# An expert tile computed at the end of attention, from counts over the first eight token tiles

## The reference

```python
def _attn_ref(q, k, v, i_gate, f_gate, o_gate):      # (4, 8, 768, 40): batch, heads, tokens, head dim
    for t in range(S):
        m_new = np.maximum(f_gate[:, :, t] + m, i_gate[:, :, t])
        f_stab, i_stab = np.exp(f_gate[:, :, t] + m - m_new), np.exp(i_gate[:, :, t] - m_new)
        m = m_new
        C = f_stab * C + i_stab * outer(v_t, k_t)
        n = f_stab * n + i_stab * k_t
        y[:, :, t] = sigmoid(o_t) * (C @ q_t) / np.maximum(np.abs(n . q_t), 1.0)

def _moe_ref(x, w_gate, w1, w2):                     # x (3072, 320); 8 experts, 320 -> 1024 -> 320
    logits = x @ w_gate
    expert_idx = np.argmax(logits, axis=1)
    gate_w = softmax(logits)[expert_idx]
    for e in range(E):
        mask = expert_idx == e
        out[mask] = gate_w[mask, None] * (np.maximum(x[mask] @ w1[e], 0.0) @ w2[e])

def _moe2_ref(x, phi, w1, w2):                       # soft mixture: 8 experts with 4 slots each
    logits = x @ phi
    slot_input = softmax(logits, over tokens).T @ x
    slot_out[e] = np.maximum(slot_input[e] @ w1[e], 0.0) @ w2[e]
    return softmax(logits, over slots) @ slot_out
```

## Time and profile before

| | |
|---|---|
| median of 3 runs | 543.53 us (543.01 to 544.75) |
| the profiled execution | 541.98 us |
| its span, first to last instruction | 540.2 us |
| mean granted TensorE clock | 0.953 of full |
| busy: TensorE, weight loads | 490.0 us (91%), 415.7 us (77%) |
| busy: VectorE, ScalarE, GpSimd | 285.9, 196.3, 327.5 us |
| DMA | 86.51 MB, 160 GB/s over the span |

### The profile page before, as it was taken

One profiled execution on the slowest core, in us unless ns is written; L12 is line 12 of the kernel. 1 busy time (PEld: TensorE's weight loads), 2 busy tenths in 40 slices (PEclk: granted clock), 3 DMA queues, 4 the chain that ended last, 5 costly groups with the idle time before them and its releaser, 6 DMA issues.

```text
span 540.2 us, 11228 instructions
## 1 busy us (share of the span) xinstructions
PE 490.0 (91%) x3957; PEld 415.7 (77%) x3957; DVE 285.9 (53%) x589; ACT 196.3 (36%) x427; POOL 327.5 (61%) x303
## 2 busy tenths in 40 slices
PE   6698999999984188999999999999999999999983
PEld 5587888888873077898989889898988988887231
DVE  7866777867784876633434444334344344334024
ACT  2544464545651402333233333233242323331013
POOL 3687878777696044569796978888098525112100
PEclk9778999989998579999999999999999999999997
DMA  8058788877930023345170505060091282106928
GB/s 226 5 166 273 268 278 254 260 245 222 304 129 36 2 71 112 99 132 218 55 247 25 226 25 227 13 239 13 27 397 33 95 345 71 53 4 259 353 108 291
DMA packets 26115, 86.51 MB, mean 160 GB/s; under 512 B 4032, under 2 KB 14384, under 8 KB 22608
## 3 DMA queue, kind: packets, MB, share of 16 engines
q1 hardware_dynamic: 19264, 75.06, 39.8%
q0 software_dynamic: 2480, 5.59, 4.0%
q10 hardware_dynamic: 4320, 5.15, 2.7%
HBM read 72.67 MB, written 8.37 MB: 150 GB/s over the span
## 4 chain that ended last, share of the span: by engine, by line
PE 47%; POOL 16%; issue 14%; DVE 11%; DMA 9%; ACT 1%; POOLq 0%; DVEq 0%; SPq 0%; ACTq 0%
DMA combine_slots<-gates,back_i 6%; PE bank L1434 5%; PE bank L1435 4%; PE bank L1436 4%; PE bank L1417 4%; PE bank L1418 4%; PE bank L1419 4%; PE bank L1445 3%; PE bank L1311 3%; DMA ys<-in_qk_columns_dram 3%; PE bank L1294 3%; POOL combine_slots L658 3%; POOL W_low L613 2%; DVE ys L948 2%; POOL hb L532 2%
## 5 line engine op out<-in xcount | busy, mean ns | idle before, releaser
L1434 PE MATMUL bank<-W_high,h_high 128*128 x248 | 79.5, 321 | 0.7 <-DVE h_low L1169 0.7
L646 POOL TENSOR_TENSOR W_high<-W,ones 128x3072 fp32r<-128x3072 f32 (+1 forms) x12 | 58.6, 4881 | 31.6 <-PE bank L1436 31.6
L1435 PE MATMUL bank<-W_high,h_low 128*128 x248 | 76.6, 309 | 0.0
L1436 PE MATMUL bank<-W_low,h_high 128*128 x248 | 76.5, 309 | 0.0
L613 POOL TENSOR_TENSOR W_low<-W,W_high 128x3072 fp32r<-128x3072 f32 (+1 forms) x12 | 75.1, 6262 | 0.9
L939 DVE RECIPROCAL hb<-hb 128x320 f32<-128x320 f32 x24 | 51.7, 2153 | 30.7 <-POOL hb L532 30.7
L828 ACT ACTIVATE h_high<-bank 128x512 fp32r<-128x512 f32 x62 | 33.7, 595 | 88.2 <-PE bank L1445 82.3
L658 POOL DMA_INDIRECT combine_slots<-gates,back_i x31 | 29.8, 961 | 54.7 <-ACT gates L808 25.7
L1154 DVE TENSOR_SCALAR hb<-bank 128x512 f32<-128x512 f32 x31 | 21.4, 691 | 77.5 <-PE bank L1421 77.5
L1417 PE MATMUL bank<-W_high,x_high 128*128 x124 | 51.9, 418 | 2.0 <-DVE x_high L1149 2.0
L1294 PE MATMUL bank<-ys 128*128 128x123 f32 (+2 forms) x384 | 50.2, 288 | 0.0
(11 more groups left out here) (270 smaller groups left out, 1069.5 us busy)
## 6 DMA issues: line engine op xcount, KB each, us to landing
W<-in_moe_w_w_dram SPq DMA_DIRECT2D x11, 1280.0 KB, 8.5
ys<-in_kvo_rows_dram SPq DMA_DIRECT2D x24, 484.0 KB, 5.7
ys<-in_qk_columns_dram SPq DMA_DIRECT2D x24, 448.0 KB, 4.7
W<-in_moe_w_w_dram SPq DMA_DIRECT2D x8, 1024.0 KB, 5.7
W<-in_moe_w_w_dram SPq DMA_DIRECT2D x2, 2560.0 KB
xs<-ys ACTq DMA_DIRECT2D x29, 160.0 KB
W<-in_moe_w_w_dram SPq DMA_DIRECT2D x9, 512.0 KB, 5.8
x_tokens<-xs SPq DMA_DIRECT2D x24, 160.0 KB, 5.2
```

What stands on the lines that cost most here:

```text
L646: g.tensor_tensor(W_high[:, columns(e % 2, part_)], w, ones[:, 0:1].broadcast_to(list(w.shape)), ALU.mult).then_inc(high_ready, 1)
L1434: mm(dst, h_high[:, kk, :], high, start=(kk == 0), stop=False)
L1435: mm(dst, h_low[:, kk, :], high, start=False, stop=False)
L1436: last = mm(dst, h_high[:, kk, :], w2_at(W_low, slot, kk), start=False, stop=(kk == NF - 1))
```

## The change

- The first steps of attention are reordered: TensorE issues scores 0, exponents 1 to 3 and scores 1 and 2 in another order with more warm-up matmuls; masking step 2's decays moves ahead of the wait for the gate columns on GpSimd; the first reciprocal stands behind the third weighing; the expansion of chunk 1 is done by VectorE.
- The load of q and k waits for the outputs only; the load of k, v and o still waits for the output gate and the state too.
- No weights are loaded before step 18. After eight steps (`EARLY`) the experts of their 1024 tokens are found (steps 13 and 14), counted (15), and the fullest ("the star") is known; by pigeonhole it has at least 128 tokens. Ranks (17), one-hots (18, 19) and slots (21) of its first 128 tokens follow, and GpSimd gathers them in step 22.
- The star's weights are loaded in step 18, all three parts at once (`expert_of(0)` is read at run time), the next expert's in step 23, a third one's after the last router. The star changes its number with expert 0, so that its tiles come first.
- Tile 0 is computed between the last attention steps: its transposes and layer 1 in steps 24 and 25, the hidden rows in 25 and 26, layer 2 behind the last logits. The loop has 30 tiles.
- ScalarE converts the star's weights in steps 19 to 21 (two, two and one pieces in place of one in each of 17 to 21); GpSimd's six pieces of the low part lie one step later.
- x is stored in the order of the steps, and the output is written in seven parts in place of five.

```diff
+        LOGITS_AT, COUNTS_AT, RANKS_AT, SLOTS_AT = EARLY + 5, EARLY + 7, EARLY + 9, EARLY + 13
...
@@ -372,20 +381,19 @@
             def load(i):
 
                 n = i % 3
+                t = tile_of_step(i)
                 if i >= 3:
                     sp.wait_ge(o_done, i - 2)
+                sp.dma_start(qkT[n][0:QROWS].rearrange("p x n t -> p (x n t)"), qk_rows[t]).then_inc(qk_in[n], 16)
+                if i >= 3:
                     sp.wait_ge(eo_ready, i - 2)
                     if i - 3 < STATES:
                         sp.wait_ge(c_done, i - 2)
-                t = tile_of_step(i)
-                sp.dma_start(qkT[n][0:QROWS].rearrange("p x n t -> p (x n t)"), qk_rows[t]).then_inc(qk_in[n], 16)
                 sp.dma_start(kvo[n], kvo_rows[t]).then_inc(kvo_in[n], 16)
...
+
+            def expert_of(n):
+                return sp.value_load(expert_at[0:1, n:n + 1], min_val=0, max_val=E - 1)
...
-                if i % 2 == 0 and i <= 20:
-                    e = (i - 4) // 6
-                    load_expert(e, e, e, parts=((i - 4) // 2 % 3,))
+                if i == 18:
+                    sp.wait_ge(order_known, 1)
+                    load_expert(expert_of(0), 0, 0)
+                if i == NT - 1:
+                    load_expert(expert_of(1), 1, 1)
             for i in range(NT - 4, NT):
                 store(i)
+            sp.wait_ge(lg_done, C)
+            sp.wait_ge(mx_tr, 1)
+            load_expert(expert_of(2), 2, 2)
...
+            mask_decays(2)
...
                     finish_x(i - 2)
-                if 0 < i and i + 1 < NT:
+                if 1 < i and i + 1 < NT:
                     mask_decays(i + 1)
                 if 1 <= i <= NT:
                     gate_times_den(i - 1)
-                if i < NT and b == 1 and c + 1 < C:
+                if B < i < NT and b == 1 and c + 1 < C:
                     expand_gates(c + 1)
...
+                if i == 22:
+                    pool.wait_ge(slots_known, 1)
+                    for n in range(3):
+                        pool.wait_ge(x_stored[n], 16 * 3)
+                    g.indirect_dma_start(first_rows[:, 0:DM], None, x_dram[0:EARLY * P, :],
+                                         bass.IndirectOffsetOnAxis(ap=slot_i[:, 0:1], axis=0)).then_inc(gath[0], 16)
+                if i > STATES:
+                    split_low_piece(i - STATES - 1)
+            split_low_piece(len(LOW_PIECES) - 1)
...
@@ -742,12 +769,24 @@
             high_parts(FIRST)
             decays(0)
             decays(1)
+            decays(2)
...
-                if 17 <= i < 17 + len(HIGH_PIECES):
-                    high_piece(i - 17)
+                if 19 <= i <= 21:
+                    for piece in ((0, 1), (2, 3), (4,))[i - 19]:
+                        high_piece(piece)
+                if i == NT:
+                    relu_low(0)
+                if i > NT:
+                    hidden_high(0, i - NT - 1, bank[6] if i == NT + 1 else bank[3])
...
-                low_parts(REST, 1).then_inc(exp_first, 1)
                 dve.wait_ge(g_tr, 1)
                 v_.tensor_copy(tdecay.rearrange("p a c h -> p (a c h)"), bank[6][:, 0:2 * C * BH])
                 v_.tensor_copy(sdecay.rearrange("p n c -> p (n c)"), bank[7][:, 0:BH // 2 * C]).then_inc(g_ready, 1)
-                dve.wait_ge(g_ready, 1)
+                low_parts(REST, 1).then_inc(exp_first, 1)
+                dve.wait_ge(exp_first, 2)
+                dve.wait_ge(g_high, 6)
+                dve.wait_ge(pads_ready, 4)
+                v_.tensor_tensor(exp_rows[1][0:HD], split_gates[0:HD, P:2 * P].unsqueeze(1).broadcast_to([HD, H, P]),
+                                 head_of[0:HD, :].unsqueeze(2).broadcast_to([HD, H, P]), ALU.mult)
+                v_.tensor_tensor(exp_cols[1][HD:P], split_gates[HD:P, P:2 * P].unsqueeze(1).broadcast_to([HD, B, P]),
+                                 batch_of[HD:P, :].unsqueeze(2).broadcast_to([HD, B, P]), ALU.mult).then_inc(exp_next, 1)
...
+            def early_choices():
+
+                dve.wait_ge(lg_copied, EARLY // B)
+                dve.wait_ge(consts, 2)
+                lgA, ohA, raA, posA = lg1[:, :, 0:EARLY], oh[:, :, 0:EARLY], ra[:, :, 0:EARLY], pos[:, 0:EARLY]
+                te = lambda a: a.rearrange("p e t -> p t e")
+                b8 = lambda a: a.unsqueeze(1).broadcast_to([P, E, EARLY])
+                e_id = col_iota[:, 0:E].unsqueeze(2).broadcast_to([P, E, EARLY])
+                ch.step(v_.tensor_reduce(mx[:, 0:EARLY], te(lgA), AX.X, ALU.max))
+                ch.step(v_.tensor_tensor(ohA, lgA, b8(mx[:, 0:EARLY]), ALU.is_ge))
+                ch.step(v_.scalar_tensor_tensor(out=raA, in0=e_id, scalar=float(-E), in1=ohA, op0=ALU.add, op1=ALU.mult))
+                v_.tensor_reduce(posA, te(raA), AX.X, ALU.min).then_inc(early_read, 1)
+
+            def early_one_hots():
+
+                ohA, posA = oh[:, :, 0:EARLY], pos[:, 0:EARLY]
+                b8 = lambda a: a.unsqueeze(1).broadcast_to([P, E, EARLY])
+                e_id = col_iota[:, 0:E].unsqueeze(2).broadcast_to([P, E, EARLY])
+                dve.wait_ge(early_read, 1)
+                ch.step(v_.scalar_tensor_tensor(out=ohA, in0=e_id, scalar=float(-E), in1=b8(posA), op0=ALU.add, op1=ALU.is_equal))
+                ch.step(v_.tensor_reduce(tiles[:, :], ohA, AX.X, ALU.add))
+                v_.tensor_copy(star_count, tiles[:, :]).then_inc(r_hot, 1)
+
+            def read_counts():
+
+                dve.wait_ge(r_rank, 1)
+                v_.tensor_copy(tiles[:, :], bank[2][:, 3 * P:3 * P + E]).then_inc(early_read, 1)
+
+            def fullest_expert():
+
+                dve.wait_ge(early_read, 2)
+                counts = tiles[:, :]
+                ch.step(v_.tensor_reduce(star_e, counts, AX.X, ALU.max))
+                ch.step(v_.tensor_tensor(tst[:, :], counts, star_e.broadcast_to([P, E]), ALU.is_ge))
+                ch.step(v_.scalar_tensor_tensor(out=tend[:, :], in0=col_iota[:, 0:E], scalar=float(-E), in1=tst[:, :],
+                                                op0=ALU.add, op1=ALU.mult))
+                ch.step(v_.tensor_reduce(star, tend[:, :], AX.X, ALU.min))
+                v_.tensor_scalar(star_hot, pos[:, 0:EARLY], star, None, ALU.is_equal).then_inc(r_hot, 1)
+                ch.step(v_.tensor_scalar(star_e, star, float(E), None, ALU.add))
+                v_.tensor_scalar(star_back, star_e, -1.0, None, ALU.mult)
+                ch.step(v_.tensor_tensor(tst[:, :], col_iota[:, 0:E], star_e.broadcast_to([P, E]), ALU.not_equal))
+                ch.step(v_.tensor_tensor(tst[:, :], tst[:, :], col_iota[:, 0:E], ALU.mult))
+                ch.step(v_.tensor_copy(tst[:, 0:1], star_e))
+                ch.step(v_.tensor_copy(expert_at[0:1, :], tst[0:1, :]))
+                dve.sem_inc(order_known, 1)
+
+            def read_ranks():
+
+                dve.wait_ge(r_rank, 2)
+                v_.tensor_copy(ra[:, 0:2, 0:EARLY], bank[2][:, 3 * P + E:3 * P + E + 2 * EARLY].rearrange("p (n t) -> p n t", n=2)).then_inc(early_read, 1)
...
+            def first_ranks():
+
+                dve.wait_ge(early_read, 3)
+                before, total = ra[:, 0, 0:EARLY], ra[:, 1, 0:EARLY]
+                rank = incl[:, 0, 0:EARLY]
+                ch.step(v_.tensor_tensor_scan(rank, ones[:, 0:EARLY], total, 0.0, ALU.mult, ALU.add))
+                ch.step(v_.tensor_tensor(rank, rank, total, ALU.subtract))
+                ch.step(v_.tensor_tensor(rank, rank, before, ALU.add))
+                ch.step(v_.scalar_tensor_tensor(out=first_of, in0=rank, scalar=1.0, in1=star_hot, op0=ALU.add, op1=ALU.mult))
+                v_.tensor_scalar(first_of, first_of, -1.0, None, ALU.add).then_inc(r_rhs, 1)
+
+            def first_hots(half_):
+
+                dve.wait_ge(r_rhs, 1 + half_)
+                for t in range(half_ * EARLY // 2, (half_ + 1) * EARLY // 2):
+                    last = v_.tensor_scalar(first_hot[:, t, :], col_iota_bf[:, :], first_of[:, t:t + 1], None, ALU.is_equal)
+                last.then_inc(r_rhs, 1)
+
+            def first_slots():
+
+                dve.wait_ge(r_slots, 1)
+                o = 3 * P + E + 2 * EARLY
+                ch.step(v_.tensor_scalar(slot_tok[:, 0:1], bank[2][:, o:o + 1], float(P), float(-P), ALU.mult, ALU.add))
+                ch.step(v_.scalar_tensor_tensor(out=slot_i[:, 0:1], in0=slot_tok[:, 0:1], scalar=0.0, in1=bank[2][:, o + 1:o + 2],
+                                                op0=ALU.max, op1=ALU.add))
+                dve.sem_inc(slots_known, 1)
...
             for i in range(NT + 2):
-                if i >= 2:
+                if i == NT:
+                    x_rest(0, 0, bank[1])
+                if i >= 3:
                     gate_reciprocal(i - 2)
                 if i < NT:
                     weigh(i)
+                if i == 2:
+                    gate_reciprocal(0)
+                if i == COUNTS_AT:
+                    read_counts()
+                if i == RANKS_AT:
```

(68 more changed lines are left out.)

305 lines of the change are left out of this document (176 added, 129 removed).

## The result

The changed kernel took 555.24 us (median of 4 executions, 554.12 to 557.66), the kernel before 543.59 beside it (543.01 to 544.75): ratio 1.0195, 95% interval 1.0153 to 1.0238. The forecast was 536.0 us and faster. The profiled execution took 554.12 us, span 552.4.

What follows compares the result with a forecast made beforehand. Bounds: a loop through several engines in attention, VectorE in routing, TensorE in the expert loop. Terms -8.8 - 1.4 - 1.8 + 0.8 + 2.3 + 0.4 + 0.8 - 0.8 + 1.0 = -7.5 us gave 536.0 us, range 532.3 to 542.3.

Steps and rivals of the forecast that it cites:

- One tile less in the loop: Expert loop: tile 0 moves to the end of attention, so one plain TensorE-bound step goes, -8.8 us.
- The start and the empty queue: Early attention: reordered first steps give -1.4 us; no weights before step 18 removes step 5's load stall, -1.8 us.
- Small operations on VectorE: Attention from step 13: 8-column operations, 0.21 us apart, partly covered by 0.88 us of idle per step, cost +2.3 us.
- The star's weights in one go: Step 18: the burst delays step 19's loads, with a margin under 1 us; +0.8 us, between 0 and +6.5.
- ScalarE's pieces: Attention steps 19 and 20: two weight conversions each where one stood, ahead of the next exponentials; +0.4 us.
- Rivals 1 and 2: Step 18 burst not hidden: 6.5 us wait, 541.7 us, chance 0.14; queue behind for four steps: 11.5 us, 546.7, 0.08.
- three signs that the prediction gave of its being wrong: Steps 19-21 over 2 us longer together; gather holding outputs 23 over 1 us; attention steps before 13 longer.
- The gather: End of attention: gather lands beside expert 1's weights, +0.8 us; layer 1 keeps TensorE's clock up, -0.8 us.
- Routing: Between attention and loop: VectorE's star number swap and an extra slot operation count in full, +1.0 us.
- rival 3: Tile 0 doesn't hide: layer 2 takes 7 us in front of the rank counts, +3.1 us, 539.1 us; chance 0.12.

Runs made afterwards that it cites:

- a_again: The kernel after, unchanged, run again in session 2: 542.25 us, ratio 1.0023 to the kernel before.
- a_two_out: The kernel after with one more wait, so that two row gathers instead of three are in flight: 559.05 us, ratio 1.0303 to the kernel before.
- m_two_out: The kernel of a_mended with at most two row gathers in flight instead of three: 556.70 us, ratio 1.0232 to the kernel before.
- b_start: The kernel before with only the reordered start and its weight parts loaded from step 8 on, no early tile: 537.97 us, ratio 0.9952 to the kernel before.
- a_counts_behind: The kernel after with TensorE's count of the eight chunks behind the outputs of chunk 14 instead of in front: 541.26 us, ratio 0.9996 to the kernel before.
- x_no_choice: The kernel after without the choice of the fullest expert (counts, product, ten of eleven small operations), expert 0 taken: 542.85 us, ratio 1.0021 to the kernel before.
- a_gather_early: The kernel after with the gather of the first tile's rows in GpSimd's step 21 instead of 22: 541.93 us, ratio 0.9991 to the kernel before.
- a_again2: The kernel after, unchanged, run again in session 3: 541.61 us, ratio 1.0027 to the kernel before.
- a_mended: The mended kernel: after with counts behind outputs, star's weights in parts over steps 17 to 19, second expert's over 20 to 22: 536.93 us, ratio 0.9925 to before.
- a_second_spread: The kernel after with only the second expert's weights in parts over steps 20 to 22: 552.45 us, ratio 1.0148 to the kernel before.
- a_again3: The kernel after, unchanged, run again in session 4: 555.34 us, ratio 1.0183 to the kernel before.

## Why the prediction was wrong

**A part of the change that got no term.** The change makes the row gathers of the loop three deep instead of two; the description of the change does not say so, and these lines are not among those shown with it (shortened with ...):

```diff
-        gath = [sem(f"gath{n}") for n in range(2)]
+        gath = [sem(f"gath{n}") for n in range(3)]
...
-                if j >= 2:
-                    pool.wait_ge(gath[n], 16 * (j // 2))
...
+                if j >= 3:
+                    pool.wait_ge(gath[j % 3], 16 * (j // 3))
```

The prediction puts this at nothing, without a reason: this is the step that failed first, and the largest. It has two prices. Three in flight: in some sessions the engines crawl and stand until 3.4 to 3.7 us after the last gather is issued, which costs 11.6 to 12.7 us over the six traces that have it. That is 12.1 of the loop's miss of 12.8 (293.94 in after, 281.83 in `a_again`), and it made the sign that was measured. Two in flight: 16.4 us in `a_two_out` and 17.1 in `m_two_out` by the gaps at tiles 6 and 9 (9.70 and 9.02 elsewhere), for GpSimd's weight parts. The gain of the tile was bound to this choice, and I looked at the gathers only for tile 0's. That three in flight is the cause is shown on the mended kernel in session 5; for the kernel after itself it is argued, from the same stall at the same place.

**One tile less in the loop, -8.8.** Right as a term: from the first matmul to the last output scaling 281.83 us in `a_again` against 289.99 before, -8.2.

**The start and the empty queue, -3.2.** Right in kind: -2.4 at weighing 12 in after, -3.4 in the trace of `b_start` and -2.7 us in its median. Weighings 5 and 6 came 5.60 us apart.

**Small operations on VectorE, +2.3.** A term that failed in attention, with its premise that only VectorE's own time counts. In steps 13 to 16 after took 27.92 us and before 24.97, +3.0, where the text had about 1.6. Of it the 2.54 us wait of TensorE for the counts was an edit whose queue I did not walk through, but `a_counts_behind` shows that removing it gives only 0.7: ScalarE comes next, 1.8 us. Nor is the term additive: `x_no_choice` took all of it out, and the time did not move.

**The star's weights in one go, +0.8, and ScalarE's pieces, +0.4.** I said that the margin was under 1 us. Steps 19 to 22 took 24.72 us against 22.40, +2.3, of which step 19 has 1.5; in other executions of the same program step 19 was 5.73. The forecast of an edge was right, and a value on an edge is no value: TensorE's wait for q and k there was 3.4 us in `a_gather_early` and 3.9 in `x_no_choice`. What sets it in one execution is not shown. Rivals 1 and 2, with waits of 6.5 us and more, did not come. Two of the three signs that the prediction gave of its being wrong did: steps 19 to 21 long by more than 2 us together (2.3), and the gather holding the outputs of step 23 by more than 1 (2.63).

**The gather, +0.8 against -0.8.** Mis-sized: +3.0. I took the 3.2 us landing of a gather that ran alone, and said that expert 1's weights would be on their way until about 162. They were issued from 156.25 on and kept the DMA engines full to about 167, and the gather, issued at 162.54, needed 5.5 us (5.7 and 6.0 in `a_again` and `a_again2`). TensorE stood 2.63 us, its granted clock was 0.67 in 168 to 170, and the outputs of step 23 took 2.95 us for the 1.92 of `a_mended`. The warm clock itself did come behind that: the last transposes took 0.55 us, where they took 0.90. `a_mended` and `a_second_spread`, which moves the second expert's weights alone, show the cause: with the same weights in parts the landing is within 3.2 us, and the wait is gone or 0.3 us. By the rule that the prediction cited from the Trainium skill ("DMA: Bandwidth & Descriptors", Queues, rings and completion order) the gather should not stand behind the weights of another queue; these traces have it 2.3 us slower beside them than in `a_mended`, so the measurement decides and the rule gave too little here.

**Routing, +1.0.** +1.8 in after, +0.2 in `a_again2`. The difference is rival 3 in small. In both traces layer 2 begins 0.55 us behind the routing's first reduction; in after its matmuls take 0.47 us each until 185.9, and VectorE waits 2.15 us for the rank counts behind it; in `a_again2` they take 0.31 us from the start and it waits 0.61, as in before. I had given this 3.1 us and 0.12.

**Without the stall** the terms come out at -8.2 for the tile, -2.4 for the start, and +9 to +12 for all that finds and feeds the tile, where I had 4.5: +9.0 makes up the trace of `a_again`, whose last output scaling is 1.6 us earlier than before's (488.38, 489.99), +11.8 its session's medians (+1.2). The likeliest reading of the change is "same" (1.0023 and 1.0027 in two sessions). Its 541.6 to 542.3 us would have lain inside the range, but by luck: the kernel before took 541.1 and 540.7 us there, so that none of the forecast gain of 7.5 us was left.

**Open.** What holds the engines in the stall, and what makes a session one with it, is not settled. The profile names no transfer or engine that TensorE waits for there, and that its instructions themselves come late is a rival that no run tests. In the sessions that had it the kernel before was slower too (543.6, 545.3 and 544.9 us, against 541.9, 541.1 and 540.7), and it is not the chip alone: sessions 1 and 4 bear the same chip number and differed, and so did sessions 3 and 5. That the kernel before with three gathers would stall wasn't tried in such a session, nor was `b_start`. That the choice of the expert is free once the loads are spread rests on one trace. Why the gathers with two in flight end 9 us later behind the loop's first matmul in `a_two_out`, `m_two_out` and one execution of `b_start` than in before is open too.

## What to carry to other kernels

- Walk through every line of a diff for its own price, above all one that changes how deep a queue is filled: here a semaphore more, in a change about something else, decided the sign.
- Where attention-like steps run with every queue nearly full, the costs of single edits don't add up; time freed on one engine goes to the next late transfer. Put large loads in parts between the small ones, ahead of the step that a gather needs, before counting instructions: the three moves of `a_mended` together brought 4.7 us, and the last of them alone 2.9 in `a_second_spread`.
- The cheap half of the change, `b_start`, gave 0.48% with two gathers in flight; it was not run in a session with the stall, and one execution of 13 lost 8 us to late weight parts. The mended kernel gave 0.75% beside it and lost 0.76% in another session: the early tile with all that feeds it was worth 1.0 us more than the start alone (536.93, 537.97).

## What the runs showed of the hardware that I had not expected

The kernel after, the same program on the same work, has two times by session: 539.8 to 545.9 us in the 22 executions of two sessions, 551.3 to 557.7 in the 10 of two others. With three indirect gathers in flight, one issued every 1.25 us for some 34 us, TensorE, VectorE and ScalarE in some sessions slow to a crawl from 224 to 232 us on and in part stand still until the gathers end; the profile names no releaser in this case ("remote", "issue"), and the DMA engines are not full (0.39 to 0.59 of their time from 230 to 242 us in after). TensorE in `a_again3`, where layer 2's matmuls start 0.15 us apart otherwise:

```profile
234.70 0.43 PE L1553 MATMUL bank<-W_high,h_high 128*128 x1 [0.99 <-issue]
236.12 0.43 PE L1554 MATMUL bank<-W_high,h_low 128*128 x1 [0.99 <-issue]
237.54 0.62 PE L1555 MATMUL bank<-W_low,h_high 128*128 x1 [0.99 <-issue]
```

In all six traces of such a stall the engines ran freely again 3.4 to 3.7 us after the last issue. With at most two in flight, the next one issued when the one two before it has landed, the two traces from such sessions (before, `m_two_out`) don't have it.

An operation on 8 columns of VectorE that takes 0.17 us elsewhere took 1.81 us in step 17 (L1115, at 130.19 us in after; 1.81 in `a_again`, `a_again2`, `a_again3` and `a_mended` too), while GpSimd ran its expansion of 64x1024 from 130.07 on; it is one of the five forecast at 0.21 us each. GpSimd's operation (1.89 us) ended at 131.96, VectorE's at 132.00. The Trainium skill ("SBUF — State Buffer", SBUF: two separate sides) says that one pair of ports is shared by these two engines and held for a whole instruction, so that the other blocks, where VectorE's operation runs in a mode that uses both its ports or has two inputs in SBUF. The trace agrees with the blocking, with the two ends 0.04 us apart; in which mode L1115 ran it doesn't show. Step 17 was 7.80 us long with it (5.65 before), of which step 18 gave 1.7 back.
